# Attention's outputs computed with columns as partitions, and the feed-forward's input loaded without transposes

## The reference

```
# attention: 4 batches, 8 heads, 768 tokens, 48 columns per head
for t in range(768):                       # a = a_re + i a_im, magnitude capped at 0.999
    S = a[t][:, None] * S + outer(k[t], v[t])   # S complex, 48 x 48 per head
    y[t] = q[t] @ real(S)
# feed-forward: x is y with the heads side by side, 3072 tokens x 384
x = ((x @ w_a) * (x @ w_b)) @ w_out        # w_a, w_b 384 x 1536; w_out 1536 x 384
# experts: each token goes to the one with the largest logit, of 8
out = gate * (relu(x @ w1[e]) @ w2[e])     # w1[e] 384 x 1024; w2[e] 1024 x 384
```

## Time and profile before

| | us |
|---|---|
| median of three runs | 1322.16 |
| profiled execution | 1323.86 |
| its span in the profile | 1321.9 |
| PE busy | 1254.0 (95%) |
| PEld busy | 1097.0 (83%) |
| DVE busy | 709.1 (54%) |
| ACT busy | 659.2 (50%) |
| POOL busy | 178.3 (13%) |

### The profile page before, as it was taken

One profiled execution on the slowest core, in us unless ns is written; L12 is line 12 of the kernel. 1 busy time (PEld: TensorE's weight loads), 2 busy tenths in 40 slices (PEclk: granted clock), 3 DMA queues, 4 the chain that ended last, 5 costly groups with the idle time before them and its releaser, 6 DMA issues.

```text
span 1321.9 us, 29322 instructions
## 1 busy us (share of the span) xinstructions
PE 1254.0 (95%) x12322; PEld 1097.0 (83%) x12322; DVE 709.1 (54%) x1032; ACT 659.2 (50%) x1236; POOL 178.3 (13%) x163
## 2 busy tenths in 40 slices
PE   6899999999999998999999999999999999999996
PEld 5888888888888887788888888888887899999996
DVE  6899999999999988411212112121123443444442
ACT  8888888888888856122222222212122444444442
POOL 1000000000000000111231322314134111111111
PEclk9999999999999999999999999999999899999998
DMA  6125556655565335400020010000002233444343
GB/s 137 38 56 151 161 167 192 184 165 151 154 168 159 117 87 213 143 0 24 1 48 1 13 36 1 24 1 24 1 7 89 71 119 128 139 138 135 135 141 117
DMA packets 198691, 126.87 MB, mean 96 GB/s; under 512 B 159388, under 2 KB 178627, under 8 KB 198576
## 3 DMA queue, kind: packets, MB, share of 16 engines
q1 hardware_dynamic: 192656, 115.43, 29.8%
q0 software_dynamic: 4352, 9.47, 2.0%
q10 hardware_dynamic: 1568, 0.30, 0.1%
HBM read 73.04 MB, written 53.70 MB: 96 GB/s over the span
## 4 chain that ended last, share of the span: by engine, by line
PE 58%; issue 1%; POOL 0%; DMA 0%; DVE 0%; ACT 0%; POOLq 0%; ACTq 0%
PE m_a L1525 12%; PE m_x L1539 11%; PE m_b L1525 11%; PE e_y L1675 10%; PE e_h L1663 10%; PE m_tr L1560 1%; PE e_tr L1633 1%; PE m_tr L1553 0%; PE m_tr L1546 0%; PE m_x L1638 0%; PE m_a L1570 0%; DMA xs_scratch<-x2s,pos 0%; DMA xe<-xs_scratch 0%; POOL xs_scratch L1320 0%; POOL out L1355 0%
## 5 line engine op out<-in xcount | busy, mean ns | idle before, releaser
L1432 DVE TENSOR_TENSOR pr<-asb,m_b 128x512 f32<-128x512 f32 x72 | 49.6, 689 | 342.4 <-ACT asb L1244 342.4
L1244 ACT COPY asb<-m_a 128x512 f32<-128x512 f32 x72 | 42.3, 588 | 349.9 <-PE m_b L1525 349.9
L885 PE MATMUL score<-QK 96*64 96x32 f32 x5376 | 180.8, 223 | 11.8 <-DVE QK L664 5.3
L885 PEld LDWEIGHTS score<-QK 96*64 96x64 f32 x5376 | 169.0, 138 | 26.1 <-DVE QK L664 10.0
L664 DVE TENSOR_TENSOR QK<-QK,E 96x1536 f32<-96x1536 f32 x80 | 140.4, 1755 | 4.1 <-PE score L885 4.1
L1332 POOL TENSOR_TENSOR pl<-pr,ph 128x512 fp32r<-128x512 f32 x71 | 92.3, 1300 | 333.9 <-ACT ph L1250 333.9
L1495 DVE SCALAR_TENSOR_TENSOR hl<-e_h,hh 128x512 fp32r<-128x512 f32 x64 | 44.3, 692 | 147.7 <-ACT hh L1287 144.1
L1663 PE MATMUL e_h<-xeh,early 128*128 128x512 f32 x384 | 119.8, 390 | 0.2 <-DVE xel L1486 0.2
L843 PE MATMUL turn<-msk,arena 128*96 128x128 f32 x576 | 85.4, 283 | 23.0 <-ACT QK L387 11.2
L843 PEld LDWEIGHTS turn<-msk,arena 128*96 128x96 f32 x576 | 56.2, 126 | 41.5 <-ACT QK L387 17.8
L1539 PE MATMUL m_x<-ph,WH 128*128 128x512 f32 x216 | 88.3, 409 | 0.6 <-POOL pl L1332 0.6
(11 more groups left out here) (247 smaller groups left out, 2880.0 us busy)
## 6 DMA issues: line engine op xcount, KB each, us to landing
xs_scratch<-zeros SPq DMA_DIRECT2D x12, 3072.0 KB, 11.3
raw<-w SPq DMA_DIRECT2D x19, 1536.0 KB, 6.7
xe<-xs_scratch SPq DMA_DIRECT2D x8, 768.0 KB, 6.4
arena<-a_re SPq DMA_DIRECT2D x32, 144.0 KB, 2.8
arena<-k SPq DMA_DIRECT2D x32, 144.0 KB, 2.8
arena<-q SPq DMA_DIRECT2D x32, 144.0 KB, 3.1
vB<-v SPq DMA_DIRECT2D x64, 72.0 KB, 2.7
x_scratch<-y_sb SPq DMA_DIRECT2D x32, 144.0 KB, 3.1
```

Of the source, the lines that this page charges most:

```text
L885: last = pe.matmul(score[n % 2][CH * g:CH * g + CH, a * HALF:(a + 1) * HALF], KT[i][0:R2, h, c * CH:(c + 1) * CH], x, start=True, stop=True)
L1244: act.copy(asb[:, n % 2, :], ap_[n % 2][:, 0:TW]).then_inc(s["a_out"], 1)
L1432: dve.tensor_tensor(pr[:, n % 2, :], asb[:, n % 2, :], bp_[n % 2][:, 0:TW], ALU.mult).then_inc(s["prod_done"], 1)
```

## The change

`outputs(u, hf)` now computes y turned: the head's columns are partitions (48, padded to 64), tokens are the free index. `hf` is the head instead of the half of the pairs. For each pair, the states are the weights (96 x 64, from `st_wide`, the padded ST, still 40 bytes apart; chunk g into partition half g) and Q moves (64 columns); then V is the weight, 128 x 128 with both column blocks, AT moves (64 columns), and the sum over 128 partitions lands in both halves. For j = 0, where chunk 0 has no state, V is used in two halves of 64 columns. vB is padded from 48 to 64 columns per block, POOL clears `st_wide` and `stl_wide` too. y_ps holds 384 columns per head instead of 288 per half; the last chunk's increments move behind them. There is one y_sb for all units instead of two, so ScalarE waits for the store of the unit before. `x_scratch` has columns as rows and tokens as columns (384 x 3072); a store is four DMAs per unit (head x chunk parity, 48 partitions each) instead of two. The feed-forward loads x as 3 x 128 columns by 512 tokens, its high and low parts are taken from SBUF, and all transposes of x go, with their waits. `zeros` is half as wide; `mx`/`v1` and `posf`/`gs` share memory, for which `gates` waits for `sorted_pos`.

```diff
@@ attention @@
-        vB = [sb(f"vB{i}", [P, 2, NC, 2, DH]) for i in both]
+        vB = [sb(f"vB{i}", [P, 2, NC, 2, CH]) for i in both]
-        ST = sb("ST", [P, 2, DH, NCH - 2])
-        STl = sb("STl", [P, 2, DH])
+        PERST = DH * (NCH - 2)
+        st_wide = sb("ST", [P, 2 * PERST + (CH - DH) * (NCH - 2)])
+        ST = st_wide[:, 0:2 * PERST].rearrange("p (h d c) -> p h d c", h=2, d=DH)
+        stl_wide = sb("STl", [P, 2 * DH + CH - DH])
+        STl = stl_wide[:, 0:2 * DH].rearrange("p (h d) -> p h d", h=2)
@@ store_y @@
                 for h in both:
-                    sp.dma_start(x_d[b + 1].rearrange("(c t) d -> t c d", t=CH)[:, :, (h0 + h) * DH:(h0 + h + 1) * DH],
-                                 y_sb[u % 2][CH * h:CH * h + CH]).then_inc(s[f"x_out{u % 2}"], 16)
+                    for g in both:
+                        sp.dma_start(x_d[(h0 + h) * DH:(h0 + h + 1) * DH, b * S:(b + 1) * S].rearrange("d (j two t) -> two d j t", two=2, t=CH)[g],
+                                     y_sb[CH * g:CH * g + DH, h].rearrange("p (j t) -> p j t", t=CH)).then_inc(s[f"x_out{u % 2}"], 16)
@@ outputs_out @@
-                if u > 1:
-                    act.wait_ge(s[f"x_out{u % 2}"], 32 * (u // 2))
-                act.copy(y_sb[u % 2][:, 6 * hf:6 * hf + 6, :].rearrange("p c d -> p (c d)"), y_ps[hf][:, 0:6 * DH]).then_inc(s["y_out"], 1)
+                if u:
+                    act.wait_ge(s[f"x_out{(u - 1) % 2}"], 64 * ((u + 1) // 2))
+                act.copy(y_sb[:, hf], y_ps[hf][:, 0:NC * CH]).then_inc(s["y_out"], 1)
@@ gpsimd @@
+            pool.memset(st_wide[:, :], 0.0)
+            pool.memset(stl_wide[:, :], 0.0)
@@ outputs @@
-                for j in range(3 * hf, 3 * hf + 3):
-                    for h in both:
-                        out = y_ps[hf][CH * h:CH * h + CH, (j - 3 * hf) * R2:(j - 3 * hf + 1) * R2]
-                        last = pe.matmul(out, AT[i][:, h * NC + j, :], vB[i][:, h, j, :, :].rearrange("p g d -> p (g d)"), start=True, stop=False)
-                        for g in both:
-                            c = 2 * j + g
-                            if c:
-                                st = ST[0:R2, h, :, c - 1] if c < NCH - 1 else STl[0:R2, h]
-                                last = pe.matmul(out[:, g * DH:(g + 1) * DH], QT[u % 2][0:R2, h, c * CH:(c + 1) * CH], st, start=False, stop=(g == 1))
+                h = hf
+                for j in range(NC):
+                    out, at = y_ps[h][:, j * CH:(j + 1) * CH], AT[i][:, h * NC + j, :]
+                    for g in both:
+                        c = 2 * j + g
+                        if c:
+                            st = h * PERST + c - 1
+                            st = st_wide[0:R2, st:st + (CH - 1) * (NCH - 2) + 1:NCH - 2] if c < NCH - 1 else stl_wide[0:R2, h * DH:h * DH + CH]
+                            pe.matmul(out[CH * g:CH * g + CH], st, QT[i][0:R2, h, c * CH:(c + 1) * CH], start=True, stop=False)
+                        else:
+                            pe.matmul(out[0:CH], vB[i][:, h, 0, 0, :], at, start=True, stop=True)
+                    if j:
+                        last = pe.matmul(out, vB[i][:, h, j, :, :].rearrange("p g d -> p (g d)"), at, start=False, stop=True)
+                    else:
+                        last = pe.matmul(out[CH:P], vB[i][:, h, 0, 1, :], at, start=False, stop=True)
@@ x_high of the feed-forward (x_low likewise) @@
-            def x_high(T, k, bank):
-                act.wait_ge(s["tr_filled"], T * KD + k + 1)
-                act.copy(xh[T % 2][:, k, :], bank[:, 0:TW]).then_inc(s["xh_done"], 1)
+            def x_high(T, k):
+                if k == 0:
+                    act.wait_ge(s[f"xin_in{T % 2}"], 16 * (T // 2) + 16)
+                act.copy(xh[T % 2][:, k, :], xin[T % 2][:, k, :]).then_inc(s["xh_done"], 1)
@@ TensorE, stage LAST + 1 (transposes of the first tile) and feed-forward step @@
-                    for k in range(KD):
-                        for c in range(TT):
-                            last = pe.transpose(x_banks[k][:, c * P:(c + 1) * P], xin0[:, c, k * P:(k + 1) * P], msk[:, 0:P])
-                        last.then_inc(s["tr_filled"], 1)
-                    if T and k < 2:
-                        pe.wait_ge(s["rt_out"], (T - 1) * TT + 3 + k)
-                    transpose_x(T + 1, k, trp)
```

More of the change, by code:

```diff
@@ L143, in attention @@
         Rw = sb("Rw", [P, 2, DH, NCH - 2])
-        ST = sb("ST", [P, 2, DH, NCH - 2])
-        STl = sb("STl", [P, 2, DH])
+        PERST = DH * (NCH - 2)
[3 more added lines that the diff above has]
+        STl = stl_wide[:, 0:2 * DH].rearrange("p (h d) -> p h d", h=2)
         AT = [sb(f"AT{i}", [P, 2 * NC, CH]) for i in both]
         KS = sb("KS", [P, 2 * NC, R2])
-        zeros = sb("zeros", [P, 2 * DM])
-        y_sb = [sb("y_sb0", [P, NCH, DH]), y_last]
+        zeros = sb("zeros", [P, DM])
+        y_sb = y_last
         used = [0]
@@ L170, in attention @@
         y_ps = [pb(f"y_ps{i}", [P, 512]) for i in both]
-        x_banks = [turn[:, 0, :], turn[:, 1, :], score[0][:, :]]
         HEAD = TOKW // 2
@@ L283, in _ @@
                     n = NE * NTOK // ZERO_PARTS
-                    sp.dma_start(xs_d[(t - 1) * n:t * n].rearrange("(n p r) c -> p n (r c)", p=P, r=2),
-                                 zeros[:, None, :].to_broadcast([P, n // (2 * P), 2 * DM])).then_inc(s["zeros_out"], 16)
+                    sp.dma_start(xs_d[(t - 1) * n:t * n].rearrange("(n p) c -> p n c", p=P),
+                                 zeros[:, None, :].to_broadcast([P, n // P, DM])).then_inc(s["zeros_out"], 16)
                 if t == ZERO_PARTS + 1:
                     for g in both:
-                        sp.wait_ge(s[f"x_out{g}"], 32 * HB)
+                        sp.wait_ge(s[f"x_out{g}"], 64 * HB)
                     for T, dst in enumerate((xin0, xin1)):
-                        row = S + T * TW
-                        sp.dma_start(dst, x_flat[row:row + TW].rearrange("(c p) d -> p c d", p=P)).then_inc(s[f"xin_in{T}"], 16)
+                        sp.dma_start(dst, x_d[:, T * TW:(T + 1) * TW].rearrange("(k p) t -> p k t", p=P)).then_inc(s[f"xin_in{T}"], 16)
                 if t + 1 == UNITS - 1:
@@ L296, in _ @@
                     load_weights(sp, mlp, arena, weights_in)
-            sp.wait_ge(s["x_out0"], 32 * (UNITS // 2))
+            sp.wait_ge(s["x_out0"], 64 * (UNITS // 2))
         @block.scalar
@@ L693, in states @@
                 ins = stt(out=STl[0:R2, h], in0=ST[0:R2, h, :, n - 1], scalar=E[LEVELS][0:R2, h, n:n + 1],
-                          in1=y_ps[0][0:R2, 6 * DH + h * DH:6 * DH + (h + 1) * DH], op0=ALU.mult, op1=ALU.add)
+                          in1=y_ps[0][0:R2, NC * CH + h * DH:NC * CH + (h + 1) * DH], op0=ALU.mult, op1=ALU.add)
                 if h == 1:
@@ L898, in increments @@
                     for j in range(NC - 1):
-                        pe.matmul(by_c[:, 2 * j:2 * j + 2, :], KS[:, h * NC + j, :], vB[i][:, h, j, :, :], start=True, stop=True)
-                    last = pe.matmul(y_ps[0][0:R2, (6 + h) * DH:(7 + h) * DH], KS[:, h * NC + NC - 1, :], vB[i][:, h, NC - 1, 0, :], start=True, stop=True)
+                        pe.matmul(by_c[:, 2 * j:2 * j + 2, :], KS[:, h * NC + j, :], vB[i][:, h, j, :, 0:DH], start=True, stop=True)
+                    last = pe.matmul(y_ps[0][0:R2, NC * CH + h * DH:NC * CH + (h + 1) * DH], KS[:, h * NC + NC - 1, :], vB[i][:, h, NC - 1, 0, 0:DH], start=True, stop=True)
                 last.then_inc(s["inc_done"], 1)
@@ L1071, in experts @@
         with ExitStack() as c1:
-            xin = [early_f[:, i * TX:(i + 1) * TX].rearrange("p (t d) -> p t d", d=DM) for i in range(2)]
+            xin = [early_f[:, i * TX:(i + 1) * TX].rearrange("p (k t) -> p k t", t=TW) for i in range(2)]
             xh, xl = ([early[:, o * TX:(o + 1) * TX].rearrange("p (k t) -> p k t", t=TW), sbt(c1, n, [P, KD, TW], F32R)] for o, n in ((2, "xh1"), (3, "xl1")))
@@ L1098, in experts @@
         s = {n: sem("e_" + n) for n in names}
-        s.update({n: earlier[n] for n in "w_high w_low xin_in0 xin_in1 tr_filled xh_done xl_done x_out0 x_out1 zeros_out".split()})
+        s.update({n: earlier[n] for n in "w_high w_low xin_in0 xin_in1 xh_done xl_done x_out0 x_out1 zeros_out".split()})
         FREE = 2
@@ L1132, in load_x @@
             def load_x(T):
-                row = S + T * TW
-                sp.dma_start(xin[T % 2][:, :, :], x_flat[row:row + TW].rearrange("(c p) d -> p c d", p=P)).then_inc(s[f"xin_in{T % 2}"], 16)
+                sp.dma_start(xin[T % 2][:, :, :], x_d[:, T * TW:(T + 1) * TW].rearrange("(k p) t -> p k t", p=P)).then_inc(s[f"xin_in{T % 2}"], 16)
             sp.dma_start(idn[:, :], ident).then_inc(s["m_const"], 16)
@@ L1157, in _ @@
             for T in range(2, TILES):
-                sp.wait_ge(s["tr_filled"], (T - 1) * KD)
+                sp.wait_ge(s["xl_done"], (T - 1) * KD)
                 if T == 2:
                     for g in range(2):
```

(18 more changed lines are left out.)

35 lines of the change are left out of this document (14 added, 21 removed).

## The result

The changed kernel takes 1465.20 us (median of four runs, 1457.48 to 1472.73), the kernel before 1322.51 in runs beside it: ratio 1.107, 95% interval 1.105 to 1.109. The forecast was 1398 us with a range to 1412, so the direction was right and the size wrong by half. The profiled execution has a span of 1462.6 us, 140.7 more than before.

The account below looks back on a forecast made before the run. Attention was taken as bound by VectorE and TensorE handing work to each other, the feed-forward by TensorE. 71.4 + 11.5 - 6.7 = +76.2; 1323.9 + 76.2 - 1.7 gives about 1398 us, range 1349 to 1412.

Parts of the forecast that it names:

- The output block at full clock: TensorE's output matmuls in an attention unit: 2.95 us before, 8.35 us after, with a load wait at each change of width.
- rival C: Output block: no load wait at the change of width, a (head, j) 0.45 us, block 5.3 us, total 1349; chance 0.11.
- The stride: Output block: state weights read 40 bytes apart cost 0.115 us per step, not 0.058, adding 1.45 us per block.
- The slack: Attention unit: the output matmuls can lengthen by 0.3 us before VectorE stands still at the level-4 update.
- Growth through 14 units: Attention units 0 to 13: block growth 5.4 us less slack 0.3, 5.1 us each, +71.4 us.
- Rival D: Attention: clock falls in part of each unit, a third of the block at half rate, 2 us a unit; chance 0.05.
- The last two units: End of attention: split outputs of unit 14 +4.8, last unit's outputs +5.4, four stores +1.3; sum +11.5 us.
- The feed-forward: Feed-forward on TensorE: 15 steps lose their four transposes of x, 0.45 us each, -6.7 us.
- Edits at nothing: Larger PSUM copies, single y_sb, four stores, POOL memsets, x loads, x parts from SBUF and the `gates` wait: all 0.

## Why the prediction was wrong

**The output block at full clock: right.** A head and pair was put at 0.76 us with strided state weights and 0.64 with ordinary ones; it took 0.75 and 0.63. The first head's part of the block lasts 166.02 - 161.97 = 4.05 us, two of them 8.1, where 8.35 was forecast. The sum charged the stride to 24 state products where the block has 20: chunk 0 adds none, and the one of the last chunk is contiguous. The wait at each change of width is there: rival C, which denied it, put a head and pair at 0.45 us and is refuted by the same rows. The groups of the weight loads say the same: in the changed kernel 15.1 us of idle time stand ahead of V's full-width loads and 12.1 us ahead of the states', with V in halves 0.0 ahead of both.

**The stride: right.** The upper bound of 0.115 us per strided step was taken against 0.058; a head and pair has two of them, and 0.75 - 0.63 = 0.12 us is what they add. With V in halves it is the same: from its first weight load to its last the block is 3.9 us long with the stride and 2.75 without in most units (85.49 - 82.74 in the timeline), about 0.06 us for each of the 20 products. A recorded weight load of ST takes 205 ns on average there with the stride and 137 without.

**The slack: right.** With V in halves the block lasts 148.28 - 144.36 = 3.92 us from its first weight load to its last, where it took 329.41 - 326.36 = 3.05 before, and the unit grew by 0.55: slack 0.32, forecast 0.3.

**Growth through 14 units: the failing step.** The prediction put a unit's growth at the block's growth less the slack, 5.1 us, and so priced the block and all that stands behind it at a granted clock of 1.00. At full clock it would be 8.1 - 2.9 - 0.3 = 4.9 us a unit (4.8 by the kernel with spares), 68 us against the 71.4 forecast. Measured are 40.30 - 30.54 = 9.8 us over 13 units and 95.32 - 87.06 = 8.3 in the first; together 619.26 - 484.03 = 135 us (VectorE's timeline of the kernel before, the updates that answer to the first and last rows above):

```profile
87.06 1.75 DVE L664 TENSOR_TENSOR QK<-QK,E 96x1536 f32<-96x1536 f32 x1
...
484.03 1.75 DVE L664 TENSOR_TENSOR QK<-QK,E 96x1536 f32<-96x1536 f32 x1
```

The other half is the clock: once it has fallen it slows the rest of the block (a head and pair in 1.05 us, not 0.75), the 48 scores behind it (2.78 us, not 1.59) and the transposes behind those (six matmuls in 1.52 us, from 174.31, not 0.86 as from 331.01 in the kernel before).

**Rival D had the fall of the clock, the wrong size and too small a chance.** It gave 0.05 to a clock that falls in part of each unit, and priced it at a third of the block at half rate, 2 us a unit. No row stood behind that length: the clock stays down 14.5 us a unit, at a cost of 9.8 - 4.9 = 4.9 us. With 4.9 in place of 2 the rival would have given 1398 + 14 x 4.9, 1467 us; this only puts the measured rest back in, it confirms nothing. The kernel before had a fall to price it by: during the last unit's outputs its clock falls to 0.50 (windows of the kernel before), and in windows of half a microsecond it stays down for 10 us.

```profile
521.00:527.00 6.00, 4.17 (x71) 4.00 (x69) 3.63 (x7) 2.94 (x5) 0.00 (x0) 0.80 0.00 0
527.00:534.00 7.00, 4.42 (x12) 3.43 (x11) 0.00 (x0) 0.40 (x1) 0.47 (x2) 0.50 0.56 118
```

An occupied TensorE is no argument against the rival: the busy share was full, 5.20 us of 5.20, in the window in which the clock fell. The runs with spare products show that what is moved counts too: with nine products of 128 moving columns the clock stays at 1.00 over ten units, with nine of 64 it is 0.82.

**The last two units: +11.5 forecast, 152.1 - 135.2 = +17 measured,** with part of them at the lower clock too (0.75 on average from 619.26 to 681.84 us). The four stores took 1.83 us of SP's time, 1.27 before.

**The feed-forward: -6.7 forecast, -11.4 measured.** The transposes gave what they should: a step that had four of them now takes 740.45 - 734.24 = 6.21 us, like its neighbours (TensorE's timeline of the kernel after, the answer to the earlier trace rows):

```profile
734.24 0.39 PE L1542 MATMUL m_x<-ph,WL 128*128 128x512 f32 x1
...
740.45 0.39 PE L1542 MATMUL m_x<-ph,WL 128*128 128x512 f32 x1
```

Of the other 4.7 us most comes from an edit costed at nothing, the shared tiles: alone they gave 3.2 us (1.9 to 5.4 by the interval). The remaining 1.5 us weren't tried by a run of their own. Of them 0.8 stand ahead of the first m_x, 544.5 - 529.73 = 14.8 us before and 695.8 - 681.84 = 14.0 after: both kernels begin the stage at the lower clock, the one before until 535, 5.3 us at 0.51, the one after until 685.5, 3.7 us at 0.52.

**Edits at nothing** otherwise held as far as a sum can tell: with V in halves and contiguous states, the single y_sb, four stores, larger copies and extra clearing are all in place, and the time is 8 us below before. None of them was tried alone.

What stays open: which property of the stream the clock follows. The length of the block alone is excluded (7.7 us of full-width products mostly keep the clock, 0.98 over ten units; 6 us with ten width changes lose it, 0.89), the stride is excluded (0.80 without it, and 1.00 with it where V is in halves), and width changes alone are excluded (the spares with 128 columns keep 1.00 beside as many of them). Waits at width changes together with few columns moved fit every run; that is a fit and was not isolated. Nor was the width of the weights tried apart from the waits: the state products have 64 columns of weights in the changed kernel and 128 in the one with everything at full width, so the two kernels differ in that as much as in their waits. Weights of 64 columns alone don't lower the clock: with V in halves all have them, at 1.00.

## What to carry to other kernels

Before fp32 products of 64 columns are given wider weights, count the full-width products that stand between narrower ones: each, with its two changes of width, made the block here 0.4 us longer than two half-width ones ((8.1 - 3.92) / 10), and ten of them cost as much again here through the clock (4.9 us a unit beside 4.9), partly outside the block and invisible in the busy share. Price a fall of the clock by how long it stays down (10 to 17 us here, once 31), not by the length of the block in which it begins. If a turned layout is wanted, take weights of one width through the block, unpadded (1316 us here, 1322 with the padding). Of the 149 us between the changed kernel and the one with 48 columns, 143 hang on the full-width load of V, as V in halves shows with the padding still there, and some 6 on the padding.

## What was not expected of the hardware

- A granted clock of 0.50 with TensorE's busy share full: 5.20 us of 5.20, and on average 14.5 us a unit.
- Added work that shortened the time: nine spare products a unit, 1465 to 1430 us; the same nine with half the columns, 1514.
- Two shared small tiles, and with them a shift of the moving operand by 32 bytes: a feed-forward step of 6.30 us became 6.18. Which of the two does it was not separated.
- Weights of 48 columns into partitions 0 to 47 and 64 to 111 run side by side like those of 64 (a V and a state product both start at 144.31 in TensorE's timeline, with 64 columns two at 147.46), and their output block is shorter: 3.3 us, with 64 columns 3.9, both with the step of 40 bytes. A stride paid by the column fits this: the recorded loads of ST last 175 ns with 48 columns and 205 with 64, those of contiguous STl 123 and 138.
